# Another order of the weight splits in the first group, with VectorE making the output weight's low parts in two blocks of three, and a prologue with its steps regrouped

## The chip, the core and the metric

One core of a Trainium2 chip runs the kernel. The metric is device microseconds, a median over executions. PE is TensorE, DVE is VectorE, ACT is ScalarE, POOL is GpSimd and SP is SyncE, which issues DMAs here.

## What is computed

Three layers in a row, in float32: a linear attention with decay over 4 batches of 768 tokens (8 heads of 48), a gated layer of width 1536, and a layer of 8 experts of width 1024 with one expert for each token.

```python
y[:, :, t] = einsum('bhd,bhde->bhe', rt, state + einsum('bhd,bhe->bhde', u * kt, vt))
state = w * state + einsum('bhd,bhe->bhde', kt, vt)
...
x = (1 / (1 + exp(-(x @ w_gate)))) * (x @ w_val) @ w_out
...
expert_idx = argmax(xn @ en.T / tau)
out[mask] = gate_w[mask, None] * (maximum(x[mask] @ w1[e], 0) @ w2[e])
```

## The kernel before

Tokens go in tiles of 128, 24 in all, and in groups of 3 tiles (G, 0 to 7, 384 tokens). A batch is six tiles, so two groups. Each engine has its own program, and semaphores tie them; an engine runs its program strictly in the order written.

**The prologue** runs attention of tiles T = 0, 1, 2 with nothing beside it. A tile has four stages. In stage 0 DVE scales k and r into kT and rT (L918, L924), and POOL makes k_tok (L575) and the product k r u in `bonus` (L582, L584, the second starts after PE has turned the tile before, because `bonus` also holds y). In stage 1 PE makes the scores (L1255, L1262), and DVE masks them and steps the state Z (L944 to L954), then sums `bonus` over a head (L957, `sum_ready`). In stage 2 PE makes y (L1278, L1286), POOL multiplies v by that sum (L588), DVE adds (L963, L969). In stage 3 PE turns y (L1292), ACT copies it to the high half `xT_hi` (L737), DVE makes the low half (L973). Beside this PE makes the logit columns of w_out^T (L1302, `logit_columns`, from the normalised expert embeddings `enT`) and, after each tile, four matmuls on a constant (L1375, `keep_clock`).

**A group** then is 12 hidden steps f (PE L1332: 18 matmuls of 128x384 for one 128-wide chunk of both gate and value), each followed by one stage of a tile of the next group, one stage for each f (f = 1 to 4 are stages 0 to 3 of T = 3, f = 5 to 8 of T = 4, f = 9 to 12 of T = 5, the last behind the first projection). After that the three projections `project` (L1353, 36 matmuls each). In each hidden step ACT takes the sigmoid (L745), DVE multiplies (L1081, `gate`), ACT makes the high half (L749) and POOL the low half of h (L618, `hlo_ready`).

**The weights** are held as a high and a low part of fp32r. In group 0 they have yet to be split: a piece (128x768; six of the gate `g`, of the value `v` and of the output weight `o`) is loaded by SP into a room, ACT writes its high part (`make_hi`, L796), and the low part is a subtraction: on DVE (`make_lo`, L1124) for g and v, on POOL (L600) for o. Hidden step f (even) of group 0 waits for the low parts of g and v number f/2. The tables `HI_AT`, `LO_AT`, `LO_O_AT` say behind which step f each is made, `PIECES` in which order and room it is loaded, and a load waits for the low part of the piece that had the room before. The third wait is in the projection: its f = 2j waits for the low part of o number j.

Of the kernel before, what the change touches and what calls it, by code (L numbers as in the profile page):

```python
# [21 lines left out]
F32 = mybir.dt.float32  # L22
# [3 lines left out]
ALU = mybir.AluOpType  # L26
# [7 lines left out]
def fused_kernel(nc, rt, kt, r, k, v, v_swap, w, u, w_gate, w_val, w_out, w_out_t, emb, tau, w1, w2, out):  # L34
# [35 lines left out]
    ROOM_OF = {(kind, j): room for kind, j, room in PIECES}  # L70
    HI_SEQ = [("g", 0), ("v", 0), ("g", 1), ("v", 1), ("g", 2), ("o", 0), ("o", 1), ("v", 2), ("o", 2), ("g", 3),
              ("v", 3), ("v", 4), ("o", 3), ("g", 4), ("o", 4), ("g", 5), ("v", 5), ("o", 5)]
    LO_SEQ = [("g", 0), ("v", 0), ("g", 1), ("v", 1), ("g", 2), ("v", 2), ("g", 3), ("v", 3), ("v", 4), ("g", 4),
              ("g", 5), ("v", 5)]
    HI_AT = {1: "g2 o0", 2: "o1 v2", 3: "o2 g3", 4: "v3", 5: "v4 o3", 6: "g4 o4", 7: "g5", 8: "v5 o5"}
    LO_AT = {0: "g1 v1", 1: "g2", 3: "v2", 4: "g3 v3", 5: "v4", 7: "g4 g5", 8: "v5"}
    LO_O_AT = {2: "o0 o1", 3: "o2", 6: "o3 o4", 8: "o5"}
    PRE, SPLIT = len(HI_SEQ), len(LO_SEQ)
    RING = 6
    assert PRE == NWO + 2 * NWG and SPLIT == 2 * NWG and EPC % 2 == 0  # L80
# [14 lines left out]
    with ctx:  # L95
# [58 lines left out]
        y = bonus[:, :, :].rearrange("p h d -> p (h d)")  # L154
        enc = A_room[0:E, 0:DM]
        bonus_sum = sb("bonus_sum", [P, H])
# [7 lines left out]
        x2 = sb("x2", [P, XW])  # L164
        row = sb("row", [P, 2, ROW])
        prio = sb("prio", [P, E])
        top = sb("top", [P, TPG, 8])
# [303 lines left out]
        def _(sp):  # L471
# [17 lines left out]

            load_pieces(PIECES[:17])  # L490
            fetch(sp, 0, 3)
            fetch_v(sp, 0, 3)
            load_pieces(PIECES[17:20])
            fetch(sp, 0, 4)
            load_pieces(PIECES[20:21])
            fetch_v(sp, 0, 4)
            load_pieces(PIECES[21:23])
            fetch(sp, 0, 5)
            fetch_v(sp, 0, 5)
            load_pieces(PIECES[23:])  # L500
# [34 lines left out]
        def _(pool):  # L535
# [55 lines left out]
            def step(b, half, G, ahead):  # L591
                for f in range(1, FC):
                    if ahead:
                        attention(*att_of(b, half, f - 1))
                    hidden_step(G, f)
                    if G == 0:
                        for kind, j in pieces_at(LO_O_AT, f):
                            _, raw, hi, lo = piece(kind, j)
                            pool.wait_ge(piece_hi, HI_SEQ.index((kind, j)) + 1)
                            g.tensor_tensor(lo, raw, hi.bitcast(F32), ALU.subtract).then_inc(piece_done_o, 1)  # L600
                if not ahead:
                    plan_constants()
# [125 lines left out]
        def _(act):  # L728
            s_ = nc.scalar

            def attention(b, c, i, stage, grp):
                T = b * TPB + c
                if stage == 3:
                    if isinstance(T, int) and T == TPG:
                        act.wait_ge(*lo_count("o", 2))
                    act.wait_ge(y_turned, T + 1)
                    s_.copy(xT_hi[:, grp, :, i * P:(i + 1) * P],  # L737
                            ps[:, BC, 0:DM].rearrange("p (c t) -> p c t", c=KC)).then_inc(xhi_ready, 1)
# [70 lines left out]
            make_hi("v", 1)  # L809
            hidden_step(0, 0)  # L810
            batches(act, step)


# [64 lines left out]
        def _(dve):  # L878
# [47 lines left out]
            def attention(b, c, i, stage, grp):  # L926
# [4 lines left out]
                elif stage == 1:  # L931
# [24 lines left out]
                    dve.wait_ge(rk_step, T * 2 + 2)  # L956
                    ve.tensor_reduce(bonus_sum[:, :], bonus[:, :, :], AX_X, ALU.add).then_inc(sum_ready, 1)  # L957
                elif stage == 2:
# [28 lines left out]
            ve.tensor_reduce(tiny[0:E, 1:2], x2[0:E, 0:DM], AX_X, ALU.add).then_inc(en_squares, 1)  # L987
            dve.wait_ge(en_norm, 1)
            link(ve.tensor_scalar(tiny[0:E, 2:3], tiny[0:E, 5:6], 1e-6, None, ALU.add))
            link(ve.tensor_tensor(tiny[0:E, 3:4], tiny[0:E, 2:3], tiny[0:E, 0:1], ALU.mult))  # L990
            link(ve.reciprocal(tiny[0:E, 4:5], tiny[0:E, 3:4]))
            ve.tensor_scalar(enc[:, :], enc[:, :], tiny[0:E, 4:5], None, ALU.mult).then_inc(en_ready, 1)
            dve.wait_ge(en_t, 1)
            ve.tensor_copy(enT[:, :, :], ps[:, BX, 0:KC * E].rearrange("p (c e) -> p c e", c=KC)).then_inc(enT_ready, 1)

# [87 lines left out]
            def step(b, half, G, ahead):  # L1083
                for f in range(1, FC):
# [3 lines left out]
                    if G == 0:  # L1088
                        for kind, j in pieces_at(LO_AT, f):
                            make_lo(kind, j)  # L1090
# [30 lines left out]
            def make_lo(kind, j):  # L1121
                _, raw, hi, lo = piece(kind, j)
                dve.wait_ge(piece_hi, HI_SEQ.index((kind, j)) + 1)
                ve.tensor_tensor(lo, raw, hi.bitcast(F32), ALU.subtract).then_inc(piece_done, 1)  # L1124

            attention(0, 0, 0, 1, 0)
            for i in range(TPG):
                if i + 1 < TPG:
                    scale_k(0, i + 1)
                    make_lo("gv"[i], 0)  # L1130
                attention(0, i, i, 2, 0)
                if i + 1 < TPG:
                    scale_r(0, i + 1)
                attention(0, i, i, 3, 0)
                if i + 1 < TPG:
                    attention(0, i + 1, i + 1, 1, 0)

# [79 lines left out]
        def _(pe):  # L1217
# [277 lines left out]
```

## Time and profile before

| | us |
|---|---|
| median of 3 runs | 878.61 (877.86 to 879.29) |
| profiled execution, its own time | 877.35 |
| its span | 875.6 |
| PE busy | 837.6 (96%) |
| DVE, POOL, ACT busy | 440.1, 423.1, 297.2 |
| mean granted TensorE clock | 0.975 |

The time lies 1.75 us around the span. PE is busy nearly throughout; what it does not fill is in the first eighth of the span, which is also where its granted clock falls below 1. A granted clock of 1.00 is 2.4 GHz and one of 0.50 is 1.2 GHz; a stretch in between is a mixture of the two.

### The profile page before, as it was taken

What the parts mean: (1) busy time and instruction counts of PE and PEld (TensorE: products, weight loads), DVE (VectorE), ACT (ScalarE), POOL (GpSimd) and SP (SyncE); (2) the same over time, 40 slices, a digit from 0 to 9 for tenths busy, and PEclk for the clock granted to TensorE, in tenths of its full rate; (3) what the DMA queues carried; (4) which work ended last, traced back from release to release, by engine and by line L of the source; (5) the groups of instructions that cost most, each with busy time, mean ns of one, the idle gap of its engine ahead of it and who ended that gap; (6) DMA issues with size and microseconds to landing.
All of it is one profiled execution on the core that took longest, in us unless ns stands there. A gap on an engine that the chain in (4) does not pass through costs nothing.

```text
span 875.6 us, 20375 instructions
## 1 busy us (share of the span) xinstructions
PE 837.6 (96%) x7466; PEld 792.2 (90%) x7467; DVE 440.1 (50%) x1051; ACT 297.2 (34%) x610; POOL 423.1 (48%) x452
## 2 busy tenths in 40 slices
PE   6778899999999999999999999998999999999995
PEld 6777899999999999999999999987999989989995
DVE  6566545545545545545545543377367267265100
ACT  1143223223223223223223214333544444454442
POOL 3465516516516516516516513336566466466544
PEclk8688899999999999999999999999999999999998
DMA  9643212212212212212212210136344354354110
GB/s 279 218 149 112 74 48 82 69 48 79 71 48 76 75 48 75 75 49 74 76 48 75 69 47 19 38 117 197 109 144 142 109 156 143 98 157 141 50 36 30
DMA packets 78421, 82.04 MB, mean 94 GB/s; under 512 B 5816, under 2 KB 75648, under 8 KB 78352
## 3 DMA queue, kind: packets, MB, share of 16 engines
q1 hardware_dynamic: 65200, 60.29, 23.1%
q10 hardware_dynamic: 9216, 9.55, 3.8%
q0 software_dynamic: 3936, 11.23, 3.4%
q8 instruction: 49, 0.80, 0.4%
q14 instruction: 20, 0.16, 0.1%
HBM read 69.83 MB, written 12.01 MB: 93 GB/s over the span
## 4 chain that ended last, share of the span: by engine, by line
PE 88%; DVE 4%; issue 2%; ACTq 2%; POOL 2%; ACT 1%; DMA 1%; POOLq 0%; DVEq 0%
PE ps L1332 33%; PE ps L1353 16%; PE ps L1435 13%; PE ps L1420 13%; PE ps L1443 3%; PE ps L1255 2%; PE ps L1278 1%; DVE weights L1124 1%; PE ps L1262 1%; PE ps L1292 1%; PE ps L1400 1%; PE ps L1286 1%; PE ps L1375 1%; ACTq L370 1%; POOL weights L600 1%
## 5 line engine op out<-in xcount | busy, mean ns | idle before, releaser
L1332 PE MATMUL ps<-x_groups,weights 128*128 128x384 f32 x1728 | 321.9, 342 | 12.2 <-DVE weights L1124 12.2
L1332 PEld LDWEIGHTS ps<-x_groups,weights 128*128 128x128 f32 x1728 | 303.3, 191 | 14.9 <-issue 13.1
L618 POOL TENSOR_TENSOR hT<-gate,hT 128x384 fp32r<-128x384 f32 x96 | 104.1, 1087 | 144.4 <-ACT hT L749 144.4
L1353 PE MATMUL ps<-weights,hT 128*128 128x392 f32 x864 | 160.6, 344 | 0.0
L1353 PEld LDWEIGHTS ps<-weights,hT 128*128 128x128 f32 x864 | 152.6, 188 | 0.4
L1435 PE MATMUL ps<-weights,hT 128*128 x672 | 124.2, 339 | 1.7 <-ACT h_f L854 1.7
L1420 PE MATMUL ps<-weights,x_groups 128*128 (+1 forms) x504 | 122.8, 397 | 1.2 <-issue 1.2
L1081 DVE TENSOR_TENSOR gate<-ps,gate 128x384 f32<-128x384 f32 x96 | 53.5, 557 | 135.4 <-PE ps L1332 129.0
L1435 PEld LDWEIGHTS ps<-weights,hT 128*128 128x128 f32 x672 | 115.9, 188 | 2.0 <-issue 1.9
L1420 PEld LDWEIGHTS ps<-weights,x_groups 128*128 128x128 f32 x504 | 92.6, 188 | 20.5 <-issue 1.7
L1067 DVE CAST weights<-staged 128x768 fp32r<-128x768 f32 x56 | 49.3, 881 | 93.5 <-PE ps L1420 54.9
L749 ACT CAST hT<-gate 128x384 fp32r<-128x384 f32 x96 | 49.3, 514 | 124.1 <-DVE gate L1081 124.1
L1069 DVE TENSOR_TENSOR weights<-staged,weights 128x768 fp32r<-128x768 f32 x60 | 80.5, 1344 | 3.5 <-ACT weights L791 1.4
L623 POOL TENSOR_TENSOR top<-top,one_half 128x1 f32<-128x1 f32 x24 | 13.5, 563 | 134.9 <-ACT row L758 134.9
L745 ACT ACTIVATE gate<-ps 128x384 f32<-128x384 f32 x96 | 47.2, 491 | 90.5 <-PE ps L1332 77.4
L704 POOL TENSOR_TENSOR hT<-h_f,hT 128x512 fp32r<-128x512 f32 x56 | 72.2, 1308 | 2.7 <-ACT h_f L854 1.8
L758 ACT ACTIVATE row<-x 128x384 f32<-128x384 f32 x24 | 12.6, 527 | 117.3 <-DVE x L1001 117.3
L836 ACT ACTIVATE A_room<-ps 128x512 f32<-128x512 f32 x56 | 33.5, 599 | 46.4 <-PE ps L1420 45.5
L688 POOL COPY dest<-Z 128x1 int32 x28 | 9.4, 336 | 74.8 <-ACT k_in L859 74.8
L859 ACT COPY k_in<-ps 128x384 f32<-128x384 f32 x28 | 13.4, 478 | 92.0 <-PE ps L1435 92.0
L692 POOL DMA_INDIRECT out<-k_in,dest x28 | 29.9, 1066 | 23.7 <-POOL dest L688 22.2
L682 POOL TENSOR_TENSOR x_groups<-kT,x_groups 128x384 fp32r<-128x384 f32 x29 | 32.9, 1134 | 16.0 <-ACT kT L831 15.9
(183 smaller groups left out, 973.0 us busy)
## 6 DMA issues: line engine op xcount, KB each, us to landing
staged<-in_moe_w SPq DMA_DIRECT2D x60, 384.0 KB, 3.4
r_in<-routed ACTq DMA_DIRECT2D x30, 192.5 KB, 2.4
rk_raw<-in_rt SPq DMA_DIRECT2D x21, 256.0 KB, 3.6
rk_raw<-in_kt SPq DMA_DIRECT2D x21, 256.0 KB, 3.9
r_in<-in_r SPq DMA_DIRECT2D x21, 192.0 KB, 2.4
k_in<-in_k SPq DMA_DIRECT2D x21, 192.0 KB, 2.5
v_in<-in_v SPq DMA_DIRECT2D x21, 192.0 KB, 2.4
A_room<-in_v_swap SPq DMA_DIRECT2D x21, 96.0 KB, 2.4
```

The source lines that it names most:

```text
L618: g.tensor_tensor(hT_lo[:, f, :], gate[:, f % 2, :], hT_hi[:, f, :].bitcast(F32), ALU.subtract).then_inc(hlo_ready, 1)
L704: g.tensor_tensor(eh_lo[:, c, :], h_f[:, c, :], eh_hi[:, c, :].bitcast(F32), ALU.subtract).then_inc(ehlo_ready, 1)
L745: s_.activation(gate[:, f % 2, :], ps[:, BG[f % 2], 0:GT], ACT.Sigmoid).then_inc(sig_ready, 1)
L749: s_.copy(hT_hi[:, f, :], gate[:, f % 2, :]).then_inc(hhi_ready, 1)
L836: s_.activation(h_rows[:, q * 512:(q + 1) * 512], ps[:, BH[q], :], ACT.Relu).then_inc(relu_ready, 1)
L1067: ve.tensor_copy(hi, raw).then_inc(ehi_step, 1)
L1069: ins = ve.tensor_tensor(lo, raw, hi.bitcast(F32), ALU.subtract)
L1081: ve.tensor_tensor(gate[:, f % 2, :], ps[:, BV[f % 2], 0:GT], gate[:, f % 2, :], ALU.mult).then_inc(h_ready, 1)
L1332: ins = te.matmul(ps[:, bank[f % 2], 0:GT], wt[:, c, fs], x[:, half, c, :], start=(c == 0 and m == 0), stop=(c == KC - 1 and m == 2))
L1353: ins = te.matmul(ps[:, BX2[i], 0:XW], h[:, f, ts], wt[:, f, :], start=(f == 0 and m == 0), stop=(f == FC - 1 and m == 2))
L1420: ins = te.matmul(ps[:, BH[q], :], x[:, c, :], columns(buf, o + c * EF + q * 512, 512), start=(c == 0 and m == 0), stop=(c == KC - 1 and m ...
L1435: ins = te.matmul(ps[:, BO, 0:DM], h[:, c, :], columns(buf, o + c * DM, DM), start=(ready is ehf_ready and c == 0 and m == 0), stop=(ready ...
```

## The change

It does four things. POOL no longer makes the low parts of the output weight; DVE does, three behind step 8 and three behind step 11. The gate and value pieces are split and loaded earlier, the output pieces later and in other rooms (s0, s1, h in place of x0, x1, x2). In the prologue DVE takes the sum of `bonus` and the low part ahead of stage 1 and not behind it, and scales the embeddings behind stage 1 of tile 0 (they move to another tile, `row`). And PE's constant matmuls behind each tile are gone, with the logit columns grouped in tiles 1 and 2. `RING` goes from 6 to 8, a count of the loads in rooms s0 and s1. `sum_bonus` and `scale_embeddings` are the lines of before as functions.

```diff
-              ("g", 3, "s0"), ("v", 3, "s1"), ("o", 0, "x0"), ("o", 1, "x1"), ("o", 2, "x2"), ("v", 4, "l3"),
-              ("g", 4, "h"), ("g", 5, "l4"), ("v", 5, "l5"), ("o", 3, "s0"), ("o", 4, "s1"), ("o", 5, "h")]
+              ("g", 3, "s0"), ("v", 3, "s1"), ("v", 4, "l3"), ("g", 4, "h"), ("g", 5, "l4"), ("v", 5, "l5"),
+              ("o", 0, "s0"), ("o", 1, "s1"), ("o", 2, "h"), ("o", 3, "s0"), ("o", 4, "s1"), ("o", 5, "h")]
...
-    HI_AT = {1: "g2 o0", 2: "o1 v2", 3: "o2 g3", 4: "v3", 5: "v4 o3", 6: "g4 o4", 7: "g5", 8: "v5 o5"}
-    LO_AT = {0: "g1 v1", 1: "g2", 3: "v2", 4: "g3 v3", 5: "v4", 7: "g4 g5", 8: "v5"}
-    LO_O_AT = {2: "o0 o1", 3: "o2", 6: "o3 o4", 8: "o5"}
+    HI_AT = {0: "g2 v2", 2: "g3", 3: "v3 v4", 4: "g4", 5: "o0 o1", 6: "g5 v5", 7: "o2", 9: "o3 o4", 10: "o5"}
+    LO_AT = {0: "g1 v1", 1: "g2 v2", 3: "g3", 4: "v3 v4", 5: "g4", 7: "g5 v5"}
+    LO_O_AT = {8: "o0 o1 o2", 11: "o3 o4 o5"}
...
-        enc = A_room[0:E, 0:DM]
+        enc = row[0:E, 1, 0:DM]
...
-            load_pieces(PIECES[:17])
+            load_pieces(PIECES[:14])
             fetch(sp, 0, 3)
             fetch_v(sp, 0, 3)
-            load_pieces(PIECES[17:20])
+            load_pieces(PIECES[14:18])
             fetch(sp, 0, 4)
-            load_pieces(PIECES[20:21])
+            load_pieces(PIECES[18:19])
             fetch_v(sp, 0, 4)
-            load_pieces(PIECES[21:23])
+            load_pieces(PIECES[19:20])
             fetch(sp, 0, 5)
+            load_pieces(PIECES[20:23])
             fetch_v(sp, 0, 5)
...
                     hidden_step(G, f)
-                    if G == 0:
-                        for kind, j in pieces_at(LO_O_AT, f):
-                            _, raw, hi, lo = piece(kind, j)
-                            pool.wait_ge(piece_hi, HI_SEQ.index((kind, j)) + 1)
-                            g.tensor_tensor(lo, raw, hi.bitcast(F32), ALU.subtract).then_inc(piece_done_o, 1)
...
-                    if isinstance(T, int) and T == TPG:
-                        act.wait_ge(*lo_count("o", 2))
...
             hidden_step(0, 0)
+            for kind, j in pieces_at(HI_AT, 0):
+                make_hi(kind, j)
             batches(act, step)
...
-                        for kind, j in pieces_at(LO_AT, f):
+                        for kind, j in pieces_at(LO_AT, f) + pieces_at(LO_O_AT, f):
                             make_lo(kind, j)
...
-                ve.tensor_tensor(lo, raw, hi.bitcast(F32), ALU.subtract).then_inc(piece_done, 1)
-
-            attention(0, 0, 0, 1, 0)
+                ve.tensor_tensor(lo, raw, hi.bitcast(F32), ALU.subtract).then_inc(lo_count(kind, j)[0], 1)
+
             for i in range(TPG):
+                if i:
+                    make_lo("gv"[i - 1], 0)
+                    sum_bonus(i)
+                attention(0, i, i, 1, 0)
+                if i == 0:
+                    sum_bonus(0)
                 if i + 1 < TPG:
                     scale_k(0, i + 1)
-                    make_lo("gv"[i], 0)
+                if i == 0:
+                    scale_embeddings()
                 attention(0, i, i, 2, 0)
                 if i + 1 < TPG:
                     scale_r(0, i + 1)
                 attention(0, i, i, 3, 0)
-                if i + 1 < TPG:
-                    attention(0, i + 1, i + 1, 1, 0)
+                if i == 0:
+                    dve.wait_ge(en_t, 1)
+                    ve.tensor_copy(enT[:, :, :], ps[:, BX, 0:KC * E].rearrange("p (c e) -> p c e", c=KC)).then_inc(enT_ready, 1)
...
             for i in range(TPG):
-                attention(0, i, i, 1)
-                if i == 0:
-                    turn_embeddings()
-                    pe.wait_ge(enT_ready, 1)
-                for c in range(4 * i, 4 * i + 2):
-                    logit_columns(c)
-                attention(0, i, i, 2)
-                for c in range(4 * i + 2, 4 * i + 4):
-                    logit_columns(c)
-                attention(0, i, i, 3)
-                keep_clock(BX2[1], 4)
+                for stage, chunks in ((1, 3), (2, 2), (3, 2)):
+                    attention(0, i, i, stage)
+                    if i == 0 and stage == 3:
+                        turn_embeddings()
+                        pe.wait_ge(enT_ready, 1)
+                    if i > 0 and (stage < 3 or i == TPG - 1):
+                        for c in range(chunk, chunk + chunks):
+                            logit_columns(c)
+                        chunk += chunks
```

DVE in the prologue, from the products of tile 1's k to its stage 2. `weights` is the low part of g0 or v0. Before:

```order
L918 TENSOR_TENSOR kT<-rk_raw,pow_k 128x512
L1124 TENSOR_TENSOR weights<-staged,weights 128x3x256
L963 TENSOR_TENSOR bonus<-ps,bonus 128x2x4x48
L969 TENSOR_TENSOR bonus<-ps,bonus 64x4x48 x2
L924 TENSOR_TENSOR rT<-rk_raw,pow_r 128x512
L973 TENSOR_TENSOR x_groups<-ps,x_groups 128x3x128
L946 TENSOR_TENSOR A_room<-ps,Z 128x192
```

and of the change:

```order
L964 TENSOR_TENSOR bonus<-ps,bonus 128x2x4x48
L970 TENSOR_TENSOR bonus<-ps,bonus 64x4x48 x2
L925 TENSOR_TENSOR rT<-rk_raw,pow_r 128x512
L974 TENSOR_TENSOR x_groups<-ps,x_groups 128x3x128
L1144 COPY enT<-ps 128x24
L1125 TENSOR_TENSOR weights<-staged,weights 128x3x256
L914 TENSOR_REDUCE bonus_sum<-bonus 128x8
L947 TENSOR_TENSOR A_room<-ps,Z 128x192
```

The low part and the sum now stand ahead of the masks of tile 1 (L947), while PE makes its scores.

POOL in hidden steps 1 to 4 of group 0, before:

```order
L618 TENSOR_TENSOR hT<-gate,hT 128x384 x2
L600 TENSOR_TENSOR weights<-group_room,weights 128x2x384 x2
L588 TENSOR_TENSOR bonus<-v_in,bonus_sum 128x384
L618 TENSOR_TENSOR hT<-gate,hT 128x384
L600 TENSOR_TENSOR weights<-group_room,weights 128x2x384
```

and DVE at the end of the hidden steps of the change, from step 8 to the entry into the projection:

```order
L1082 TENSOR_TENSOR gate<-ps,gate 128x384
L974 TENSOR_TENSOR x_groups<-ps,x_groups 128x3x128
L1125 TENSOR_TENSOR weights<-staged,weights 128x2x384 x2
L1125 TENSOR_TENSOR weights<-h_f,weights 128x2x384
L1082 TENSOR_TENSOR gate<-ps,gate 128x384
L919 TENSOR_TENSOR kT<-rk_raw,pow_k 128x512
L925 TENSOR_TENSOR rT<-rk_raw,pow_r 128x512
L1082 TENSOR_TENSOR gate<-ps,gate 128x384
```

POOL's v-product (L588) no longer has two low parts ahead of it; DVE has three between the gate of step 8 and that of step 9, with kT and rT of T = 5 behind them.

## Rows read from the trace of the kernel before

**Rows 1.** The page: TensorE's costliest group, with its idle time before it.
```profile
L1332 PE MATMUL ps<-x_groups,weights 128*128 128x384 f32 x1728 | 321.9, 342 | 12.2 <-DVE weights L1124 12.2
```
**Rows 2.** Busy by stretch: us, PE, PEld, DVE, ACT, POOL; clock, DMA, GB/s.
```profile
44.10:108.70 64.60, 52.18 (x592) 49.40 (x590) 37.85 (x52) 22.59 (x41) 38.64 (x29) 0.87 0.37 112
...
130.00:400.00 270.00, 270.00 (x2867) 260.15 (x2866) 141.88 (x436) 79.57 (x173) 122.66 (x123) 1.00 0.22 65
```
**Rows 3.** PE's timeline: start, us, what, and idle before with its releaser.
```profile
66.89 5.46 PE L1332 MATMUL ps<-x_groups,weights 128*128 128x384 f32 x18 [5.80 <-DVE weights L1124]
...
77.39 3.39 PE L1332 MATMUL ps<-x_groups,weights 128*128 128x384 f32 x18 [1.58 <-DVE weights L1124]
...
90.83 5.44 PE L1332 MATMUL ps<-x_groups,weights 128*128 128x384 f32 x18 [4.57 <-DVE weights L1124]
```
**Rows 4.** The chain of waits into the 66.89 step: start, us, what.
```profile
58.70 3.73 POOL weights L600 x2
...
64.58 2.18 DVE weights L1124
```
**Rows 5.** The chain of waits through tiles 1 and 2 and hidden step 0.
```profile
23.68 1.71 PE ps L1375 x8
...
27.32 0.36 DVE A_room L946
...
28.87 0.46 DVE bonus_sum L957
...
31.36 0.56 DVE bonus L963
...
32.62 0.90 PE ps L1292 x3
33.53 1.71 PE ps L1375 x8
...
42.40 1.71 PE ps L1375 x8
44.11 4.78 PE ps L1332 x18
```
**Rows 6.** The timelines of PE, DVE and POOL in the prologue.
```profile
14.56 0.63 PE L1262 MATMUL ps<-v_in,k_tok 64*64 64x48 f32 x32
...
17.48 0.35 DVE L944 COPY A_room<-ps 128x192 f32<-128x192 f32 x1
...
24.83 0.99 POOL L584 TENSOR_TENSOR bonus<-bonus,u_tok 128x384 f32<-128x384 f32 x1
...
28.97 0.68 PE L1278 MATMUL ps<-first_room,A_room 64*64 64x48 f32 x32 [0.93 <-DVE A_room L935]
...
30.05 1.12 PE L1302 MATMUL ps<-enT,group_room 128*64 128x8 f32 x24
```
**Rows 7.** The timelines of DVE and POOL, 49 to 57 us.
```profile
49.45 0.95 DVE L1124 TENSOR_TENSOR weights<-h_f,weights 128x768 fp32r<-128x768 f32 x1
...
54.46 1.34 POOL L584 TENSOR_TENSOR bonus<-bonus,u_tok 128x384 f32<-128x384 f32 x1
...
54.85 1.76 DVE L1124 TENSOR_TENSOR weights<-first_room,weights 128x768 fp32r<-128x768 f32 x1
```
**Rows 8.** DMA issues, the last load of tile 2, issued at 17.20: KB, us to landing.
```profile
first_room<-in_v_swap ACTq DMA_DIRECT2D x1, 96.0 KB, 12.3
```
**Rows 9.** The timelines of DVE and PE around stage 2 of T = 3 and kT, rT of T = 5.
```profile
58.20 0.75 DVE L954 TENSOR_TENSOR Z<-Z,w_pow 128x192 f32<-128x192 f32 x1
...
59.94 0.26 PE L1278 MATMUL ps<-v_in,A_room 64*64 64x48 f32 x2
...
97.15 0.56 DVE L973 TENSOR_TENSOR x_groups<-ps,x_groups 128x384 fp32r<-128x384 f32 x1 [0.21 <-ACT x_groups L737]
...
101.62 1.50 DVE L924 TENSOR_TENSOR rT<-rk_raw,pow_r 128x512 f32<-128x512 f32 x1
```
**Rows 10.** Busy by stretch, columns as in rows 2: a stretch of the prologue.
```profile
20.00:30.00 10.00, 8.00 (x199) 7.50 (x194) 6.46 (x15) 1.63 (x3) 5.65 (x7) 0.66 1.08 347
```

More of the change, by code:

```diff
@@ L67, in fused_kernel @@
               ("t", 4, "x1"), ("t", 5, "x2"), ("g", 1, "h"), ("v", 1, "l3"), ("g", 2, "l4"), ("v", 2, "l5"),
[2 rows of a table removed]
[2 rows of a table added]
     ROOM_OF = {(kind, j): room for kind, j, room in PIECES}
-    HI_SEQ = [("g", 0), ("v", 0), ("g", 1), ("v", 1), ("g", 2), ("o", 0), ("o", 1), ("v", 2), ("o", 2), ("g", 3),
-              ("v", 3), ("v", 4), ("o", 3), ("g", 4), ("o", 4), ("g", 5), ("v", 5), ("o", 5)]
+    HI_SEQ = [("g", 0), ("v", 0), ("g", 1), ("v", 1), ("g", 2), ("v", 2), ("g", 3), ("v", 3), ("v", 4), ("g", 4),
+              ("o", 0), ("o", 1), ("g", 5), ("v", 5), ("o", 2), ("o", 3), ("o", 4), ("o", 5)]
     LO_SEQ = [("g", 0), ("v", 0), ("g", 1), ("v", 1), ("g", 2), ("v", 2), ("g", 3), ("v", 3), ("v", 4), ("g", 4),
               ("g", 5), ("v", 5)]
-    HI_AT = {1: "g2 o0", 2: "o1 v2", 3: "o2 g3", 4: "v3", 5: "v4 o3", 6: "g4 o4", 7: "g5", 8: "v5 o5"}
-    LO_AT = {0: "g1 v1", 1: "g2", 3: "v2", 4: "g3 v3", 5: "v4", 7: "g4 g5", 8: "v5"}
-    LO_O_AT = {2: "o0 o1", 3: "o2", 6: "o3 o4", 8: "o5"}
+    HI_AT = {0: "g2 v2", 2: "g3", 3: "v3 v4", 4: "g4", 5: "o0 o1", 6: "g5 v5", 7: "o2", 9: "o3 o4", 10: "o5"}
+    LO_AT = {0: "g1 v1", 1: "g2 v2", 3: "g3", 4: "v3 v4", 5: "g4", 7: "g5 v5"}
+    LO_O_AT = {8: "o0 o1 o2", 11: "o3 o4 o5"}
     PRE, SPLIT = len(HI_SEQ), len(LO_SEQ)
-    RING = 6
+    RING = 8
     assert PRE == NWO + 2 * NWG and SPLIT == 2 * NWG and EPC % 2 == 0
@@ L913, in _, with sum_bonus @@
             w128 = w_pow[:, 7, :]
+            def sum_bonus(T):
+                dve.wait_ge(rk_step, T * 2 + 2)
+                ve.tensor_reduce(bonus_sum[:, :], bonus[:, :, :], AX_X, ALU.add).then_inc(sum_ready, 1)
             def scale_k(b, c):
@@ L955, in attention @@
                                          ALU.mult).then_inc(z_ready, 1)
-                    dve.wait_ge(rk_step, T * 2 + 2)
-                    ve.tensor_reduce(bonus_sum[:, :], bonus[:, :, :], AX_X, ALU.add).then_inc(sum_ready, 1)
+                    if not isinstance(T, int) or T >= TPG:
+                        sum_bonus(T)
                 elif stage == 2:
@@ L987, in _, with scale_embeddings @@
             ve.tensor_reduce(tiny[0:E, 1:2], x2[0:E, 0:DM], AX_X, ALU.add).then_inc(en_squares, 1)
[L988 to L994, printed above, removed]
+            def scale_embeddings():
+                dve.wait_ge(en_norm, 1)
+                link(ve.tensor_scalar(tiny[0:E, 2:3], tiny[0:E, 5:6], 1e-6, None, ALU.add))
+                link(ve.tensor_tensor(tiny[0:E, 3:4], tiny[0:E, 2:3], tiny[0:E, 0:1], ALU.mult))
+                link(ve.reciprocal(tiny[0:E, 4:5], tiny[0:E, 3:4]))
+                ve.tensor_scalar(enc[:, :], enc[:, :], tiny[0:E, 4:5], None, ALU.mult).then_inc(en_ready, 1)
             def choose(G, i):
@@ L1380, in _ @@
             keep_clock(BC, 8)
+            chunk = 0
             for i in range(TPG):
-                attention(0, i, i, 1)
-                if i == 0:
-                    turn_embeddings()
-                    pe.wait_ge(enT_ready, 1)
-                for c in range(4 * i, 4 * i + 2):
-                    logit_columns(c)
-                attention(0, i, i, 2)
-                for c in range(4 * i + 2, 4 * i + 4):
-                    logit_columns(c)
-                attention(0, i, i, 3)
-                keep_clock(BX2[1], 4)
+                for stage, chunks in ((1, 3), (2, 2), (3, 2)):
[7 more added lines that the diff above has]
+                        chunk += chunks
+            assert chunk == FC
             hidden_step(0, 0, 0, first=True)
```

## The prediction

> **What bounds the kernel now.** I read the page's costliest groups first. TensorE's hidden matmuls wait 12.2 us in all, always for a low part on VectorE [rows 1]. Then the busy time by stretch: from 44.1 to 108.7 us, the twelve hidden steps of group 0, PE is busy 52.18 of 64.60 us at a clock of 0.87, while from 130 to 400 us it is busy all the time at 1.00 [rows 2]. So the loss lies in group 0 and in the prologue ahead of it, and what is saved there should reach the end whole: behind it there is no idle time to fall into.
>
> PE's timeline names the waits: 5.80 us ahead of step 4, 1.58 ahead of step 6, 4.57 ahead of step 8 [rows 3]; 12.2 less these leaves 0.25 for step 2. The steps behind the two long waits take 5.46 and 5.44 us, that behind the short one 3.39 [rows 3]: after the long waits the granted clock is at 1.2 GHz for a step. The chain says where the first wait is from: POOL makes two low parts of the output weight, 3.73 us, POOL's v-product stands behind them, DVE's y-sum waits for that, and the low part of v2, which PE waits for, stands behind the y-sum (begun at 64.58) and takes 2.18 [rows 4]. Step 8 repeats it a tile later. In the prologue the chain runs through DVE's instructions in series and through a burst of 1.71 us of constant matmuls after every tile [rows 5].
>
> **The prologue: minus 4.7 us.** Tile 0: scores are out at 15.2 (14.56 + 0.63), but DVE takes them up at 17.48, behind the scaling of the embeddings [rows 6]. In the change it takes them at 15.2. The four small instructions come behind the sum, in the way of the y-sum, and ACT's first high part (its wait stood in the old chain) no longer does. Counting on from 15.2 with masks and decay 1.7, sum 0.5, kT 0.6, the four 1.6, y-sum 1.2 and turn 0.9, the turn ends at 21.7 and not at 23.68: minus 2.0.
>
> Tiles 1 and 2 I measure from one turn's end to the next, now 9.85 (23.68 to 33.53) and 8.87 (to 42.40) [rows 5]. In the change POOL's two products of `bonus` come first after the turn, 0.99 each [rows 6], with DVE's low part of 0.95 between them, since the two take turns (below), then the sum 0.46 [rows 5]: 3.4 with the handovers. Masks and decay take 1.55 (27.32 to 28.87), PE's stage 2 about 1.1 (28.97 to the next work at 30.05) [rows 6], the y-sum 1.26 (31.36 to 32.62), the turn 0.90 [rows 5]: together 8.3. The sum and the low part no longer stand between the masks and the y-sum, and the burst is gone. Turns end at 30.0 and 38.3, in place of 33.53 and 42.40. The inputs allow it: tile 2's last load lands at 29.5 (17.20 + 12.3) [rows 8], 0.5 before PE asks. Behind the last turn ACT's and DVE's halves of x take 1.1 us, so hidden step 0 starts at 39.4, where it stood at 44.11 behind the burst [rows 5]: minus 4.7. The twelve logit chunks cost nothing: PE does them while it waits for DVE in tiles 1 and 2, the last two in that 1.1.
>
> **The old waits: minus 12.2, and the cold steps: minus 4.2.** The POOL low parts are gone, so its v-product runs as soon as the sum is there. Further, g2 and v2 are split behind step 1 for step 4, g3, v3 behind steps 3 and 4 for step 6, g4 behind 5 for step 8, g5 and v5 behind 7 for step 10: the waits of [rows 3] came from low parts made in the one or two steps before. The loads allow it: g2 to v3 are in before the stage, v4 and g4 go out behind the low parts of v1 and g1, three steps before ACT wants them. With the waits go the two slow steps, 5.46 + 5.44 less twice 3.37, which is 4.2 [rows 3].
>
> **What the low parts cost on DVE: 3.5 us of new waits.** Alone a low part takes 0.95 us. One that meets POOL's work took 1.76: it is begun at 54.85, POOL's product ends at 55.80, and 0.81 later the low part ends [rows 7]. So the two do not share; one stands until the other's instruction is over. The Trainium skill (SBUF — State Buffer, section SBUF: two separate sides) says that of a VectorE instruction with two SBUF inputs and a GpSimd one the first takes the port pair for its whole length; this trace agrees, with the 0.81. DVE has 37.85 us in the stage [rows 2]; three more low parts in it (the other three come in the projection) at 0.95 to 1.76 make 41 to 43 of about 52, so it has room on the average, and what counts is the place.
> Place one: behind step 1 there are two low parts where there was one, so the gate of step 2 and the decay of T = 3 come up to 1.9 later (1.76, or an instruction more on POOL). The decay ended at 58.95 and PE took it up at 59.94 [rows 9], a slack of 1.0: I take 1.2 of wait, after a trial count with POOL's turns, between 0.8 and 1.3.
> Place two: the block of three behind step 8. Before, from the end of x's low half to rT of T = 5 was 5.4 us (97.71 to 103.12) [rows 9]. Now it is 0.95 + 2 x 1.76 for the block, 0.5 for the gate, 2.6 for kT and rT: 7.6. PE needs 6.74 for steps 9 and 10 and the block starts 1.1 into step 9, so stage 1 waits 1.1 + 7.6 - 6.74 = 2.0. With 0.3 at other places (stage 1 of T = 4 and the handovers) the new waits sum to 3.5.
> Place three: the block behind step 11 runs with projection 0, which wants o3 half-way through. Counted at 0.95 each it is a microsecond early; three at 1.76 would be up to 1.4 late. I take nothing, and 1.4 for the range.
>
> Hidden step 0 took 4.78 with the clock rising in it [rows 5]; after the change fewer matmuls go before it, and I put it at the cold 5.45: plus 0.7.
>
> **Sum:** -4.7 - 12.2 - 4.2 + 3.5 + 0.7 = -16.9 us. The profiled execution would go from 877.35 to 860.5. Its time lies 1.26 under the median of the runs; against that median the forecast is 878.6 - 16.9 = 861.7. Bounds of the terms: with no new wait -20.4, and with the prologue a half microsecond better -20.9, which is 857.7.
>
> **The rivals.**
> A. *The clock falls again.* The waits of 1.2 and 2.0 lie beside stages of small matmuls. For it: 4.57 of waiting was enough. Against: step 6, after 1.58, ran in 3.39 [rows 3]; 2.0 is nearer to that. Each fall costs 2.1, so 863.8 or 865.9.
> B. *DVE becomes the bound of the stage.* Every low part and every kT and rT meets POOL's work. DVE at 43 us of 52 leaves little, and the third place adds its 1.4; with 3 more at the first two, 866. The Trainium skill (Perfetto Trace Analysis, Optimizing Scalar/DVE Operations) advises moving work off a saturated DVE, even to GpSimd, and warns that the shared port may take the gain; this change goes the other way. Here DVE was busy 37.85 of 64.60 us [rows 2], which is not saturated.
> C. *The prologue is held by its loads.* Tile 2's v lands only 0.5 before it is wanted; two us later in landing would leave 2.7 of the 4.7, that is 863.7.
> D. *Slower: the clock stays at 1.2 GHz.* The bursts may hold what clock there is. If it stays low through the hidden steps, twelve steps at 5.45 and 7 us of attention stages end at 39.4 + 72.5 = 111.9, in place of 108.7, and the waits hide in it: 881.8 or more. It decides from eight cold steps on (16.9 over 2.08). Against it: with the bursts the clock was 0.66 anyway from 20 to 30 us [rows 10], and it rose within step 0. The Trainium skill (TensorE: Matmul & The Clock Gate, section What's actually happening) has the throttled state as the default that activity releases, which speaks against taking matmuls away; by it alone the steps come warm a little into steady work, as step 0 did.
> E. *No change* (within 0.2%, 1.8 us, about what a measurement of this kernel can tell): only if DVE gave all of it back.
>
> **Chances:** the forecast 0.58, A 0.18, B 0.11, C 0.08, D 0.03, E 0.02. The faster cases make 0.95, the same 0.02, slower 0.03. The range reaches down to the bound without new waits, 857.5, and up over A twice, B and C to 868.
>
> **What the changed profile would show.** Hidden step 0 starting near 39.4; no PE wait on a low part in group 0; instead about 1 us ahead of stage 2 of T = 3 (for the decay) and 2 ahead of stage 1 of T = 5 (for rT); steps at 3.4 from step 1 or 2 on; the first projection near 92. I am wrong if steps of 5.4 appear in the middle of the stage, if PE waits for the gate or for low parts of the output weight in projection 0, or if the later stretches are no longer full.

## The result, and the profile after

The change takes 868.68 us (median of 4 runs, 868.17 to 868.93) where the kernel before, on the same chip, took 878.95 (4 runs, 877.86 to 879.74): ratio 0.9883, 95% interval 0.9866 to 0.9900. It is faster by 10.3 us. The forecast was 861.7 with a range to 868.0, so the sign came out, and the mechanism in the hidden steps, and the size did not: 7 us of the gain are missing. The profiled execution took 868.17 with a span of 866.4, against 877.35 and 875.6 before.

The page of the change: instructions, the busy and clock rows in 40 slices, and PE's two costliest groups with their idle time before.

```profile
span 866.4 us, 20325 instructions
...
PE   5999899999999999999999999989999999999995
...
PEclk8599999999999999999999999999999999999999
...
L1340 PE MATMUL ps<-x_groups,weights 128*128 128x384 f32 x1728 | 319.5, 341 | 0.2 <-DVE weights L1125 0.2
...
L1361 PE MATMUL ps<-weights,hT 128*128 128x392 f32 x864 | 160.6, 344 | 0.0
```

The first group had 12.2 us of waiting on low parts [rows 1] and has 0.2. The projections (L1361) wait for nothing. But the second digit of the clock is a 5. What PE waits for now, from hidden step 0 to projection 0 (us in total, times, longest):

```profile
PE ps L1263 <- DVE rT L925: 3.9, 2, 2.8
PE ps L1286 <- DVE A_room L936: 0.7, 1, 0.7
PE ps L1340 <- DVE weights L1125: 0.2, 1, 0.2
```

Busy by stretch, columns as in [rows 2]. The second row covers the stage, the counterpart of the first row of [rows 2]; the first row stands against [rows 10].

```profile
20.00:30.00 10.00, 8.09 (x184) 7.42 (x185) 6.60 (x16) 1.17 (x2) 5.37 (x5) 0.50 1.08 348
...
42.30:97.20 54.90, 50.03 (x592) 47.55 (x590) 42.29 (x57) 23.09 (x41) 29.05 (x23) 0.93 0.44 134
```

From 20 us to hidden step 0 the clock is 0.50, which is 1.2 GHz throughout; from 20 to 30 us it was 0.66 before. The stage is 54.9 us long in place of 64.6. The chain of waits gives the places (start, us, what): tiles 1 and 2, hidden step 0, and the end of the stage.

```profile
21.07 0.92 PE ps L1300 x3
...
25.19 2.02 PE ps L1310 x36
27.21 1.04 PE ps L1286 x32
28.25 0.85 PE ps L1294 x32
29.10 0.95 PE ps L1310 x14
...
30.25 0.71 PE ps L1310 x7
30.96 0.85 PE ps L1300 x3
...
36.76 1.10 PE ps L1286 x32
37.87 0.85 PE ps L1294 x32
...
40.97 1.39 PE ps L1310 x24
42.35 5.42 PE ps L1340 x18
...
91.30 4.90 PE ps L1340 x18
...
97.27 2.87 PE ps L1361 x15
```

The change term by term, in us of the profiled executions:

| term | forecast | measured |
|---|---|---|
| prologue, to hidden step 0 (44.11 to 42.35) | -4.7 | -1.8 |
| old waits, 12.2 to 0.2 | -12.2 | -12.0 |
| the two slow steps, now 3.4 each | -4.2 | -4.2 |
| new waits, 0.72 + 1.08 + 2.83 | +3.5 | +4.6 |
| hidden step 0, 4.78 to 5.42 | +0.7 | +0.6 |
| a new slow step, 4.90 for 3.37 | 0 | +1.5 |
| left over in the stage | 0 | -0.2 |
| behind projection 0's start | 0 | +2.3 |
| sum | -16.9 | -9.2 |

The last row but one is 875.6 - 108.73 = 766.9 before and 866.4 - 97.27 = 769.1 after. The medians differ by 10.3 and the two profiled executions by 9.2, because that of before lies further under its median.

### The profile page after: what moved, and what is told of

Read it like the earlier page. It is cut to its first block, busy times and chain, and to the rows that moved or that the text cites. A ratio compares the mean times of both kernels' runs of the same rounds, so it can differ in the third digit from the quotient of the medians.

```text
span 866.4 us, 20325 instructions
## 1 busy us (share of the span) xinstructions
PE 835.3 (96%) x7442; PEld 789.6 (91%) x7443; DVE 448.5 (52%) x1057; ACT 297.5 (34%) x610; POOL 415.4 (48%) x446
## 4 chain that ended last, share of the span: by engine, by line
PE 93%; DVE 4%; issue 1%; POOL 1%; DMA 0%; ACT 0%; SPq 0%; POOLq 0%; ACTq 0%; DVEq 0%
PE ps L1340 34%; PE ps L1361 18%; PE ps L1443 14%; PE ps L1428 13%; PE ps L1451 3%; PE ps L1286 2%; PE ps L1263 2%; PE ps L1383 2%; PE ps L1294 1%; PE ps L1270 1%; PE ps L1300 1%; PE ps L1408 1%; DVE weights L1125 1%; PE ps L1310 1%; DMA w_col<-in_w 0%
## 5 line engine op out<-in xcount | busy, mean ns | idle before, releaser
L1340 PE MATMUL ps<-x_groups,weights 128*128 128x384 f32 x1728 | 319.5, 341 | 0.2 <-DVE weights L1125 0.2
L1340 PEld LDWEIGHTS ps<-x_groups,weights 128*128 128x128 f32 x1728 | 301.1, 190 | 2.6 <-issue 0.5
L614 POOL TENSOR_TENSOR hT<-gate,hT 128x384 fp32r<-128x384 f32 x96 | 104.5, 1091 | 144.7 <-ACT hT L743 144.7
L1361 PE MATMUL ps<-weights,hT 128*128 128x392 f32 x864 | 160.6, 344 | 0.0
L1361 PEld LDWEIGHTS ps<-weights,hT 128*128 128x128 f32 x864 | 152.6, 188 | 0.4
L1070 DVE TENSOR_TENSOR weights<-staged,weights 128x768 fp32r<-128x768 f32 x60 | 83.3, 1392 | 3.5 <-ACT weights L785 1.4
```

The lines of the kernel that those rows point to most:

```text
L614: g.tensor_tensor(hT_lo[:, f, :], gate[:, f % 2, :], hT_hi[:, f, :].bitcast(F32), ALU.subtract).then_inc(hlo_ready, 1)
L1070: ins = ve.tensor_tensor(lo, raw, hi.bitcast(F32), ALU.subtract)
L1340: ins = te.matmul(ps[:, bank[f % 2], 0:GT], wt[:, c, fs], x[:, half, c, :], start=(c == 0 and m == 0), stop=(c == KC - 1 and m == 2))
L1361: ins = te.matmul(ps[:, BX2[i], 0:XW], h[:, f, ts], wt[:, f, :], start=(f == 0 and m == 0), stop=(f == FC - 1 and m == 2))
```

## Experiments

Twelve runs were made: eleven other kernels, and the change once more. In every one I read the same marks: where hidden step 0 and projection 0 start by PE's timeline (the chain puts both up to 0.4 us later), the length of the stage between them, and the span.

| kernel | step 0 | stage | projection 0 | span | median | ratio to before |
|---|---|---|---|---|---|---|
| before | 43.8 | 64.9 | 108.7 | 875.6 | 878.95 | |
| change | 42.3 | 54.9 | 97.2 | 866.4 | 868.68 | 0.9883 (0.9866 to 0.9900) |
| change again | 42.5 | 54.6 | 97.1 | 866.3 | 868.34 | 0.9902 (0.9876 to 0.9929) |
| stage_only | 43.6 | 54.5 | 98.1 | 866.2 | 867.76 | 0.9893 (0.9868 to 0.9918) |
| prologue_only | 42.6 | 64.8 | 107.4 | 875.4 | 877.83 | 1.0015 (1.0002 to 1.0028) |
| bursts | 47.0 | 55.4 | 102.3 | 869.7 | 870.31 | 0.9914 (0.9882 to 0.9946) |
| spread | 43.0 | 50.2 | 93.2 | 861.1 | 862.20 | 0.9833 (0.9804 to 0.9861) |
| fill | 43.3 | 54.5 | 97.8 | 867.2 | 868.29 | 0.9899 (0.9873 to 0.9924) |
| pool_low | 42.6 | 57.4 | 100.0 | 870.4 | 871.12 | 0.9924 (0.9895 to 0.9953) |
| sum_late | 40.9 | 55.0 | 95.9 | 864.9 | 866.92 | 0.9883 (0.9855 to 0.9911) |
| spread_o | 43.2 | 51.5 | 94.7 | 862.5 | 864.27 | 0.9850 (0.9825 to 0.9874) |
| both | 41.6 | 49.9 | 91.5 | 859.8 | 860.93 | 0.9808 (0.9780 to 0.9836) |
| both_ent | 40.2 | 50.0 | 90.2 | 859.2 | 860.89 | 0.9819 (0.9786 to 0.9851) |
| both_warm | 41.4 | 47.1 | 88.5 | 858.1 | 860.68 | 0.9817 (0.9779 to 0.9856) |

They ran in three sets. Before took 876.84 on the chip of stage_only, prologue_only, bursts and spread, 877.53 on that of change again, fill, pool_low and sum_late, and 878.09 on that of the last four. Between sets the ratios are to be compared, not the times. Edits that add or remove lines move the line numbers by a few: L1338 is L1340 of the change.

### Which half brought the gain

**stage_only** is the change with the prologue of before: on PE the loop with `keep_clock`, on DVE the old order.

```diff
-                for stage, chunks in ((1, 3), (2, 2), (3, 2)):
...
+                attention(0, i, i, 3)
+                keep_clock(BX2[1], 4)
```

> The change with the prologue of before (order of DVE's steps, logit columns, a burst of constant matmuls behind each tile). Theory 1: the prologue's part of the gain is only 1.8 us, since hidden step 0 began at 42.35 and not at 39.4; the hidden steps of group 0 give the rest. Then hidden step 0 is back at 44.1, the stage from there to the projection is 54.9 as in the change (53.4 if the clock does not fall in it), and the time is 869 to 870.5. Rival: the new prologue also helps or harms the stage (clock, loads), then the stage differs from 54.9 by over 2 and the time lies outside 868 to 871.5.

**prologue_only** is the kernel before with the prologue of the change; tables, loads and POOL's low parts are those of before.

> The change's prologue with the split tables, the loads and POOL's low parts of before. Theory 1: hidden step 0 at 42.3, then the three waits of before (5.8, 1.6, 4.6) and both cold steps are back: 877 (1.8 under before). Rival: the waits before were partly due to the old prologue and shrink with it: 874 or less.

stage_only has the whole gain: 0.9893, within the interval of the change, and 1.2 us under the lower end of what was expected. prologue_only has none: 1.0015, where a time 1.8 us under before was expected, and although its step 0 starts 1.2 us earlier. Its interval (1.0002 to 1.0028) lies just above 1. So the gain comes from the hidden steps, that is from the tables, the loads and the engine of the output weight's low parts together, and the new prologue is worth nothing that the time shows. Where its 1.2 us go is open: its profiled span is 875.4 us, that of before 875.6.

### The prologue: bursts, or a clock that is low

**bursts** puts the constant matmuls behind each tile back into the change.

```diff
                             logit_columns(c)
                         chunk += chunks
+                keep_clock(BX2[1], 4)
```

> The change with the burst of four constant matmuls behind each tile put back, nothing else. Theory 1 (the prologue lost 2.9 of its 4.7 us because PE ran at 1.2 GHz all through it, stage 2 taking 1.9 us where it took 1.1): the bursts cost 1.7 each but bring the clock up for stretches between them, so stage 2 of some tile is back at 1.1 and the time stays within 1.5 us of the change, 868 to 870.5. Rival (the clock did not matter, DVE and POOL taking turns did): stage 2 stays at 1.9 and each burst on the path adds its 1.7, 871.5 to 873.5.

The median, 870.31, is 2.5 us above stage_only on the same chip (the intervals of the ratio overlap), and step 0 starts 4.7 later than in the change. The chain of waits of this kernel around tile 1's burst, and its busy time by stretch:

```profile
33.32 0.83 PE ps L1300 x3
34.15 1.71 PE ps L1383 x8
35.86 1.06 PE ps L1263 x32
```

```profile
20.00:30.00 10.00, 7.82 (x134) 7.02 (x138) 6.47 (x14) 1.98 (x4) 5.45 (x5) 0.50 1.08 349
30.00:40.00 10.00, 9.78 (x203) 9.23 (x199) 5.41 (x12) 0.48 (x1) 3.50 (x3) 0.50 0.35 103
```

A burst stands on the path with its full 1.71 us, and up to step 0 it buys no clock: 0.50 with it as without it, and the scores still take 1.06 us (L1263). The time fell within the expected 868 to 870.5, but not for the reason expected: stage 2 stayed at 1.9 to 2.0 us. What the bursts do give back is in step 0, which takes 4.13 us here and 5.42 in the change. They cost more than that on the path of the prologue; whether the total time is longer, the overlapping intervals do not decide. Taking them away was not what lowered the clock.

**fill** puts constant matmuls where PE waits in tile 0, off the path.

```diff
                     attention(0, i, i, stage)
+                    if i == 0 and stage < 3:
+                        keep_clock(BX2[1], (4, 6)[stage - 1])
```

> The change with constant matmuls put where PE stands idle in tile 0 (4 behind its scores, 6 behind its stage 2), off the path of DVE. Theory (the lost 2.9 us of the prologue are the clock of 1.2 GHz): the clock holds at 2.4 through tile 0 into tile 1, whose scores and stage 2 take 1.3 and 1.1 in place of 1.96 and 1.9, so hidden step 0 comes 0.7 to 2 us earlier: 40.3 to 41.6. Rival (DVE and POOL in turns set the pace, PE's speed does not matter): hidden step 0 within 0.3 of 42.3.

The clock was 1.00 from 12 to 20 us and 0.65 in the next ten, where the change had 0.76 and 0.50, and then 0.50 again. It was up only to about 22.5 us: PE then waited 2.32 us for the turned embeddings, and tile 1's scores and stage 2 took as long as in the change. A gap of 0.83 us inside that stage 2, in which PE waited for nothing that the profile shows, comes on top. Step 0 starts at 43.3, 0.8 later than in the change again and not earlier as expected, and the median is the change's. Filling the gaps of tile 0 doesn't carry over the next two, so this kernel does not test what the prologue would take with the clock up.

**sum_late** leaves DVE's sum of `bonus` behind the masks in every tile.

```diff
                 if i:
                     make_lo("gv"[i - 1], 0)
-                    sum_bonus(i)
                 attention(0, i, i, 1, 0)
-                if i == 0:
-                    sum_bonus(0)
+                sum_bonus(i)
```

> The change with DVE's sum of bonus behind the masks again in tiles 1 and 2, not ahead of them. Theory: the masks waited 1.3 us a tile for POOL's two products and the sum (3.3 us from the turn's end, when the scores were there after 2.0), so masks come 1.3 earlier, stage 2 by 0.7 (the three logit columns, 2.0 us at 1.2 GHz, then stand ahead of it), and hidden step 0 comes 1 to 2 us earlier: 40.3 to 41.3. Rival (PE's small work at 1.2 GHz is the chain): within 0.3 of 42.3.

Step 0 came 1.6 us earlier than in the change again, and the median fell by 1.4 (the two intervals of the ratio overlap; the marks of the trace do not leave it open). In the change the masks of tile 2 (`A_room` L947) stand in the chain behind two POOL products and the sum:

```profile
31.88 1.00 POOL bonus L583
...
32.95 1.68 POOL bonus L585
...
34.66 0.55 DVE bonus_sum L914
35.21 0.26 DVE A_room L947
```

PE's scores of this tile end at 33.7 us; it then makes logit columns and waits another 1.06 us for the masks and what DVE makes of them, none of which needs the sum. With the sum behind them PE's chain is without a gap from 30.00 to step 0. So this part of the change, which I had costed as a gain, is a loss of 1.6 us in the prologue.

### The stage: the block of three

**spread_o** takes the block of three behind step 8 apart.

```diff
-    LO_O_AT = {8: "o0 o1 o2", 11: "o3 o4 o5"}
+    LO_O_AT = {8: "o0", 10: "o1 o2", 11: "o3 o4 o5"}
```

The high parts of o3 to o5 go behind steps 10 and 11 with it, and one v load goes ahead of the last three pieces.

> Only the output weight's part of the experiment spread (one low part behind step 8, two behind 10, loads reordered); the gate and value tables are the change's. Theory: the 2.8 us ahead of stage 1 of T = 5 and the slow step after it go, the 1.1 ahead of stage 1 of T = 4 stays: stage from hidden step 0 to the projection 54.8 less 3.5 to 4.3, that is 50.5 to 51.3, time 864 to 865. Rival (the gate and value tables of spread did most): stage 53 or more.

**spread** does the same and also takes the pairs of gate and value parts apart.

```diff
-    LO_AT = {0: "g1 v1", 1: "g2 v2", 3: "g3", 4: "v3 v4", 5: "g4", 7: "g5 v5"}
+    LO_AT = {0: "g1 v1", 1: "g2", 2: "v2", 3: "g3", 4: "v3", 6: "v4 g4", 7: "g5 v5"}
```

> The change with the output weight's first low parts not in one block behind step 8 (one behind 8, two behind 10), v2, v4, g4 a step or two later, and the loads of v for T = 5 ahead of the fourth output piece. Theory: the 2.8 us wait ahead of stage 1 of T = 5 is that block, three low parts taking turns with POOL's four instructions there, and the clock's fall after it follows from that wait; so wait and fall go (-2.8 -1.5), and the 1.1 ahead of stage 1 of T = 4 too: 863 to 864.5. Rival: DVE has no room anywhere in the stage, the wait appears elsewhere (in the projection, for o4 or o5): 866.5 to 869.

DVE and POOL in the change, around the block (timelines: start, us, what, idle before):

```profile
82.10 3.50 DVE L1125 TENSOR_TENSOR weights<-staged,weights 128x768 fp32r<-128x768 f32 x2
85.52 1.77 DVE L1125 TENSOR_TENSOR weights<-h_f,weights 128x768 fp32r<-128x768 f32 x1
```

```profile
82.08 1.01 POOL L614 TENSOR_TENSOR hT<-gate,hT 128x384 fp32r<-128x384 f32 x1 [3.43 <-ACT hT L743]
83.05 1.73 POOL L576 TENSOR_TENSOR k_tok<-k_in,pow_tok 128x384 f32<-128x384 f32 x1
84.75 1.73 POOL L583 TENSOR_TENSOR bonus<-k_in,r_in 128x384 f32<-128x384 f32 x1
86.56 1.59 POOL L585 TENSOR_TENSOR bonus<-bonus,u_tok 128x384 f32<-128x384 f32 x1
```

Each of the three low parts meets an instruction of POOL: the first the low part of h (L614), the second k_tok, the third the first product of `bonus`. So each takes about 1.75 and the block 5.2 us. PE then waits 2.83 for rT, and step 11 takes 4.90. In spread the waits of PE on rT are one of 0.8:

```profile
PE ps L1263 <- DVE rT L925: 0.8, 1, 0.8
```

and no step behind step 0 is slow. In spread_o the longest wait is 1.1 and step 11 is not slow either. The stage of spread is 50.2 us long, against 54.6, and 51.5 in spread_o, which keeps the wait at T = 4. The ratio goes from 0.9902 to 0.9833 and 0.9850. The block of three, with the slow step behind it, thus costs 3.1 us in the stage, and the pairs another 1.3; between spread and spread_o the intervals of the ratio overlap, and the marks of the trace tell them apart.

### The order, or the engine

**pool_low** keeps the change's tables but lets POOL make the output weight's low parts, behind the same steps.

```diff
-                        for kind, j in pieces_at(LO_AT, f) + pieces_at(LO_O_AT, f):
+                        for kind, j in pieces_at(LO_AT, f):
```

> The change with the output weight's low parts back on POOL, in the same two blocks of three behind steps 8 and 11. Theory 1 (order and place did it, the engine matters less): the three old waits stay away; behind step 8 POOL has 5.5 us of low parts ahead of k_tok of T = 5, so PE waits for that at stage 1 of T = 5, 2 to 5 us, and the second block (5.5 us at 1.8 each) is late in projection 0 by up to 2: 868 to 873. Rival (moving the work to DVE is the gain): the old waits of 4 to 6 us come back and it lies above 875.

It is still 6.4 us faster than before and 2.8 slower than the change. The old waits stay away, so it is the new order and places of the splits and loads that remove them, and not the engine. The waits of PE, us in total:

```profile
PE ps L1275 <- DMA A_room<-in_v_swap: 3.4, 1, 3.4
PE ps L1268 <- DVE rT L930: 1.5, 2, 1.1
PE ps L1366 <- POOL weights L601: 0.8, 2, 0.4
```

and its chain of waits shows why a load is late:

```profile
83.38 4.11 POOL weights L601 x2
...
87.50 0.37 SPq L488
...
88.42 3.60 DMA A_room<-in_v_swap
...
92.16 1.09 PE ps L1275 x16
93.25 5.71 PE ps L1345 x18
```

SP's load of an output piece waits for a low part on POOL, and the v of T = 5 is queued behind that on SP. VectorE is through with the second of these parts at 85.6 us, POOL at 87.5, and with VectorE the wait doesn't arise. By the medians about two thirds of the change's gain is the order and one third the engine. The intervals of the two ratios overlap, and VectorE with the old tables was not tried, so this share is rough.

### Together

**change again** is the change, for the same chip as the second set.

> The change itself once more, on the same chip as the next three. Theory: hidden step 0 at 42.3, the stage from there to the projection 54.9. Between the last projection and the first expert matmul the change took 15.6 us where before and the other kernels took 13.1 to 13.7, with the clock at 1.2 GHz for a stretch; if that is a matter of when the clock looks, another profile may have 13.2 there, and the span is 864; if it belongs to this kernel, 15.6 and 866.4 again.

Its stage and marks repeat. What doesn't is the handover, below. It takes 13.9 us here and not 15.6, as in the first of the two cases expected, but the span is 866.3 as in the second: from the first expert matmul to the end it is 280.4 us here and 278.7 in the change.

**both** is spread with sum_late.

> spread and sum_late together. Theory: the gains are in different stretches and add up: hidden step 0 at 40.9, stage 50.2, projection at 91.1, time 860.5 to 862. Rival: an earlier stage meets loads that have not landed (g3, v3 are loaded behind the low parts of g0 and v0), and some of it comes back as a wait in the stage: projection at 92.5 or later.

It takes 860.93, ratio 0.9808: its interval lies under that of the change, and it beats the kernel before by 17 us and the change by 7 to 8. Its longest wait in the stage is 0.6 us, on rT of T = 5.

**both_ent** also copies `enT` ahead of x's low half in tile 0, which frees PE's stage 1 of tile 1 sooner.

```diff
+                if i == 0:
+                    dve.wait_ge(en_t, 1)
+                    ve.tensor_copy(enT[:, :, :], ...
                 attention(0, i, i, 3, 0)
```

> both, with the turned embeddings copied ahead of x's low half of tile 0. Theory: PE waited 0.8 to 1.1 us for that copy before tile 1's scores, so hidden step 0 comes 0.5 to 0.9 earlier, near 40.2. Rival: tile 2's last load (lands at 29.5) holds tile 2 and nothing is gained.

Step 0 starts 1.4 us earlier, the span is 0.6 shorter, and the median is the same (860.89). Part of it comes back as a wait of 0.54 us inside projection 0 for the last low part of the output weight, whose high part is not there earlier (DVE waits 1.79 us for it); both has no such wait.

**both_warm** is both_ent with constant matmuls nearly everywhere: 9 and 12 in the calls of tile 0's stages 1 and 2, and 3 behind the turned embeddings and behind the logit columns of stages 1 and 2.

> both_ent with constant matmuls in every gap of PE in the prologue (9 and 12 in tile 0, 3 behind the turned embeddings, 3 behind each block of logit columns of stages 1 and 2). Theory (PE at 1.2 GHz in tiles 1 and 2 costs 2 us or more): the clock stays at 2.4 GHz, scores take 1.3, stage 2 1.1, the turn 0.35, and hidden step 0 comes at 38 to 39.5 with its first step below 4. Rival: the clock falls anyway, or what it gives is what the matmuls cost, and hidden step 0 is not before 40.

Its busy time by stretch, and its chain of waits in tile 2 and before it:

```profile
20.00:30.00 10.00, 7.89 (x198) 7.07 (x198) 6.05 (x16) 1.45 (x3) 5.75 (x5) 0.87 1.08 348
30.00:40.00 10.00, 9.87 (x236) 9.16 (x235) 6.37 (x15) 0.48 (x1) 3.51 (x3) 0.79 0.43 126
```

```profile
26.47 2.11 issue
...
31.27 1.58 PE ps L1381 x6
...
37.02 0.68 PE ps L1284 x32
37.71 0.47 PE ps L1292 x32
...
41.44 3.39 PE ps L1338 x18
```

The clock is up, stage 2 takes 1.15 us where it took 1.95, and step 0 takes 3.39. But the bursts that make it so stand on the path themselves, and a gap of 2.11 us appears inside stage 2 of tile 1 in which PE waits for nothing that the profile shows. Projection 0 starts 1.7 earlier than in both_ent, the wait inside it is 1.10 us, and the median is the same within its interval (860.68). With enough constant work the clock can be had in the prologue; in this kernel what it costs is about what it gives.

## Why the prediction was right or wrong

**What bounds the kernel: right up to the experts.** From the start of projection 0 to the constant matmuls ahead of the experts it is 474.97 us before and 474.98 in the change, and what group 0 saves arrives there whole. That it would reach the end whole did not hold in the profiled executions (the tail, below).

**"The old waits: minus 12.2, and the cold steps: minus 4.2": right.** 12.0 and 4.2 measured. pool_low shows that the earlier splits do this, whichever engine makes the output weight's low parts.

**"The prologue: minus 4.7 us": failed, by 2.9.** Tile 0's end was right, 21.99 for 21.7, but in part by luck: DVE took the scores up at 13.73 and not at 15.2, and the sum then waited 0.89 us for POOL's product, an input that I had not counted there; the four small instructions took 2.1 and not 1.6. The step that failed is "PE's stage 2 about 1.1" together with "the twelve logit chunks cost nothing". The 1.1 came from a row with the clock up, 0.68 us for L1278 [rows 6]. At the 0.50 of the changed prologue stage 2 takes 1.04 + 0.85 and 1.10 + 0.85: 0.8 more in each of two tiles. The logit columns are longer too, 2.02 us for three chunks, and hold stage 2 by 0.3, the turn of tile 1 by 0.5 and step 0 by 0.3. Together that is 2.7. I had changed what PE does around these rows and priced what was left by rows of the old arrangement. That this sizes the miss is read from the durations; what lowered the clock is not shown. The Trainium skill (TensorE: Matmul & The Clock Gate, section What's actually happening) has the low clock as the default, released by activity. The fall from 0.66 to 0.50 agrees with it in direction. But bursts, with the constant matmuls back behind the tiles, also shows 0.50, and fill, with some in tile 0, shows 0.65 from 20 to 30 us, so their number alone doesn't decide it here.

And the sum ahead of the masks was no gain: I costed it as moved out of the way of the y-sum, and did not ask what POOL's two products cost in front of it. sum_late has that at 1.4 to 1.6 us.

**"What the low parts cost on DVE: 3.5 us of new waits": mis-sized, 4.6, and 6.1 with what follows.** Place one: 0.72 for 1.2. Stage 1 of T = 4, inside the "0.3 at other places": 1.08, since the low parts of v3 and v4 both met POOL and took 1.81 and 1.76. Place two: 2.83 for 2.0. I wrote the block as 0.95 + 2 x 1.76 (4.5) and it took 5.2, because POOL had three instructions ready and not two. That port rule (the Trainium skill, SBUF — State Buffer, section SBUF: two separate sides) held for all 13 low parts of the stage. The nine that met an instruction of POOL took 1.7 to 1.8 us, the four that met none 0.9 to 1.0, so it should have been applied to every low part. Place three was right: 98.60 for two in 1.83 and one in 0.95, and no wait in the projection. DVE's 42.29 us in the stage is within the 41 to 43.

**Rival A (0.18) happened, once.** Behind the wait of 2.83 step 11 took 4.90: plus 1.5, forecast 2.1. Behind 0.72 and 1.08 the steps stayed at 3.3. I had argued that 2.0 is nearer to 1.58 than to 4.57. The wait came out 0.8 longer; whether 2.0 would have been short enough no run shows. Behind the same wait of 2.8 the slow step took 4.43 (fill), 4.53 (change again, stage_only), 4.90 (sum_late) and 5.53 us (bursts), so the price of one is 1.1 to 2.2. spread and spread_o, with waits of 1.1 at most, have no slow step behind step 0.

**Rival B** did not decide: DVE has room on the average. B's mechanism, that the low parts meet POOL, held in places one and two and not in place three. **Rival C** did not happen; no wait of PE in tile 2 is on a load. **Rival D** was wrong about the steps, which ran at 3.4 from step 1 on, but half right about the prologue: its clock did stay at 1.2 GHz. **Rival E** fell.

**What no term had: plus 2.3 behind projection 0.** It lies at the handover to the experts. PE's timeline there before, in the change, and in the change again:

```profile
583.63 8.28 PE L1375 MATMUL ps<-ident 128*128 128x128 f32 x72
593.42 0.55 PE L1400 MATMUL ps<-ident,r_in 128*128 128x128 f32 x3 [1.50 <-DMA r_in<-routed]
```

```profile
572.18 9.91 PE L1383 MATMUL ps<-ident 128*128 128x128 f32 x72
583.28 0.55 PE L1408 MATMUL ps<-ident,r_in 128*128 128x128 f32 x3 [1.18 <-issue]
```

```profile
572.06 8.28 PE L1383 MATMUL ps<-ident 128*128 128x128 f32 x72
581.93 0.55 PE L1408 MATMUL ps<-ident,r_in 128*128 128x128 f32 x3 [1.59 <-DMA r_in<-routed]
```

In the change the 72 constant matmuls took 9.91 us, at a mean clock of 0.83. In the change again they took 8.28, as before the change, and yet the rest of the span is as long. That kernel has gaps of 0.38 us behind them and 1.30 ahead of a matmul of the expert layer, in which PE waits for nothing that the profile shows. From the constant matmuls to the end before has 292.0 us and the thirteen others have 292.4 to 294.5. prologue_only, which is the old stage, has 293.0. So part of the 2.3, about 1.0, may be that the one profiled execution of before was short there. Why the rest differs from kernel to kernel was not tried and stays open.

Summed: of the 7.7 us by which the profiled gain fell short, 2.9 is the prologue at the low clock, 1.1 the new waits, 1.5 the slow step behind the longest of them, 2.3 the tail; small differences of the other terms cancel. Projection 0 starts at 97.2 and not near 92. Two sums of the prediction are off without weight: the terms of tiles 1 and 2 add up to 8.2 and not 8.3 each, and the lower bound is 857.7 by its own sum, where the range has 857.5.

## What to carry to other kernels

Price every small instruction that is to run beside another engine's stream on the shared port at the locked price (here 1.76 and not 0.95 us for 128x768), and put such work in ones and twos between the things that others wait for; three in a row cost 3 us that one and two did not. When work is taken away from TensorE, look first at the granted clock of the rows that price what remains. And ask of an instruction that is moved earlier what it waits for: a sum put ahead of masks waits for its own inputs, and so then do the masks. Last, a start made earlier is worth only what the next wait leaves of it: in both_ent 1.4 us in the prologue brought 0.6 in the span and nothing in the median.

## What was not expected of the hardware

- The clock of a prologue of small matmuls. PE was busy 8.09 of 10 us with them at 0.50, and 9.78 of 10 in bursts, also at 0.50. In both_warm it was busy 7.89 of 10 at 0.87. The busy share of such stretches does not tell the clock.
- Gaps in which PE waits for nothing that the profile shows, in the middle of a run of matmuls: 2.11 us inside a stage 2 in both_warm, 0.83 inside one in fill, 1.18 at the handover of the change. They differ between executions of the same kernel: at the handover's first place the change again has 1.59 us, and there the profile names the load of the routed rows. The 0.7 us ahead of stage 2 of T = 3 is none of them, though the profile names nothing in front of it in spread_o: DVE's decay of that tile ends at 61.00 us and PE starts at 61.10, as with 59.51 and 59.62 in the change.
- The price of a slow step. A wait of 2.8 us was followed by steps of 4.43 to 5.53 us in six kernels with the same tables, where waits of 4.57 and 5.80 were followed by 5.44 and 5.46 [rows 3]: the slow time is not a fixed price, and the length of the wait alone does not set it.
